# The second half of an MLP group, moved ahead of the transposes in the attention steps

## The reference, cut to what matters

```python
# attention: q, k, v are (4, 8, 576, 64)
scores = scale * np.matmul(q, k.transpose(0, 1, 3, 2))
mask = block_i >= block_j                      # blocks of 64 positions
scores = np.where(mask, scores, -1000000000.0)
scores = scores - np.max(scores, axis=-1, keepdims=True)
attn = np.exp(scores)
attn = attn / (np.sum(attn, axis=-1, keepdims=True) + 1e-09)
out = np.matmul(attn, v)
...
# dense MLP: x is (2304, 512), w_in (512, 2048), w_out (2048, 512)
h = x @ w_in
g = np.maximum(0.01 * h, h)
return (g @ w_out).astype(np.float32)
...
# routed MLP: 8 experts of 512 x 1024 and 1024 x 512, one for each token, and a skip
```

## Time and profile before

| what | value |
|---|---|
| three runs | 756.45, 757.16, 758.13 us; median 757.16 |
| the profiled execution | 757.67 us, of which the span of the trace is 755.9 |
| TensorE busy | 739.1 us, 98% |
| its weight loads busy | 595.1 us, 79% |
| Vector, Scalar, POOL engine busy | 360.1, 296.7, 146.0 us |
| chain that ended last | 92% PE, 3% DMA, 2% ACT, 2% DVE |

### The profile page before, as it was taken

How to read it: one execution, slowest core, us unless ns; L and a number is a source line. 1 busy time by engine, 2 the same in 40 slices (tenths; PEclk the granted TensorE clock), 3 DMA queues, 4 the chain that set the end, 5 groups by cost and what they waited for, 6 DMA issues and landing times.

```text
span 755.9 us, 12647 instructions
## 1 busy us (share of the span) xinstructions
PE 739.1 (98%) x4358; PEld 595.1 (79%) x4359; DVE 360.1 (48%) x761; ACT 296.7 (39%) x674; POOL 146.0 (19%) x190
## 2 busy tenths in 40 slices
PE   7999999999999999999999999999999999999997
PEld 4556777788877887797888788888787879999984
DVE  5777554465446442013435465555655352352641
ACT  5567565455445543234423222132221131342550
POOL 3136565233222221100020000000000032212221
PEclk9999999999999999999999999999999999999999
DMA  4345777545554522546756566666653117777771
GB/s 128 98 125 164 209 207 224 150 132 151 145 163 140 145 85 72 149 134 166 216 180 187 160 181 165 199 166 177 184 157 99 57 40 249 230 235 245 234 235 56
DMA packets 97537, 121.60 MB, mean 161 GB/s; under 512 B 13842, under 2 KB 60706, under 8 KB 97480
## 3 DMA queue, kind: packets, MB, share of 16 engines
q1 hardware_dynamic: 94664, 116.50, 52.8%
q0 software_dynamic: 1920, 3.77, 1.5%
q10 hardware_dynamic: 896, 0.59, 0.2%
HBM read 89.09 MB, written 31.31 MB: 159 GB/s over the span
## 4 chain that ended last, share of the span: by engine, by line
PE 92%; DMA 3%; ACT 2%; DVE 2%; issue 2%; POOL 0%; SPq 0%; DVEq 0%; POOLq 0%; ACTq 0%
PE ps_x L1809 9%; PE ps_x L1811 9%; PE ps_x L1810 9%; PE ps_h L1727 9%; PE ps_hid L1981 9%; PE ps_h L1729 8%; PE ps_h L1728 8%; PE ps_o L1710 6%; PE ps_t L1684 5%; PE ps_y L1992 2%; PE ps_y L1994 2%; PE ps_y L1993 2%; PE ps_s L1635 2%; PE ps_s L1672 2%; PE ps_s L1671 2%
## 5 line engine op out<-in xcount | busy, mean ns | idle before, releaser
L1727 PE MATMUL ps_h<-xh,win_h 128*128 128x512 f32 (+1 forms) x320 | 124.3, 388 | 5.1 <-ACT act L1083 4.9
L1729 PE MATMUL ps_h<-xh,win_l 128*128 128x512 f32 (+1 forms) x320 | 118.4, 370 | 0.0
L1728 PE MATMUL ps_h<-xl,win_h 128*128 128x512 f32 (+1 forms) x320 | 118.1, 369 | 0.0
L1809 PE MATMUL ps_x<-wout_h,g_hi 128*128 128x512 f32 x288 | 114.0, 396 | 0.0
L1811 PE MATMUL ps_x<-wout_h,g_lo 128*128 128x512 f32 x288 | 112.3, 390 | 0.0
L1810 PE MATMUL ps_x<-wout_l,g_hi 128*128 128x512 f32 x288 | 112.1, 389 | 0.0
L1069 ACT ACTIVATE prob<-ps_s,neg_max 128x128 f32<-128x128 f32 (+3 forms) x144 | 79.0, 550 | 59.5 <-DVE neg_max L1290 42.5
L1290 DVE TENSOR_REDUCE neg_max<-ps_s 128x1 f32<-128x128 f32 (+3 forms) x144 | 71.1, 509 | 58.0 <-PE ps_s L1672 36.2
L1083 ACT ACTIVATE act<-ps_h 128x512 f32<-128x512 f32 (+1 forms) x80 | 44.3, 554 | 106.3 <-PE ps_h L1729 100.0
L1330 DVE TENSOR_TENSOR g_lo<-g_raw,g_hi 128x512 fp32r<-128x512 f32 x72 | 49.5, 687 | 66.9 <-ACT g_hi L1093 66.8
L1727 PEld LDWEIGHTS ps_h<-xh,win_h 128*128 128x128 f32 x320 | 60.3, 189 | 18.2 <-issue 4.7
(11 more groups left out here) (205 smaller groups left out, 1098.5 us busy)
## 6 DMA issues: line engine op xcount, KB each, us to landing
g_raw<-hidden SPq DMA_DIRECT2D x72, 256.0 KB, 3.9
hidden<-act SPq DMA_DIRECT2D x64, 256.0 KB, 2.6
w_sb<-in_w SPq DMA_DIRECT2D x32, 512.0 KB, 5.0
w_two<-in_w SPq DMA_DIRECT2D x32, 512.0 KB, 4.6
k_raw<-in_k_t SPq DMA_DIRECT2D x40, 144.0 KB, 3.1
x2rows<-x SPq DMA_DIRECT2D x18, 256.0 KB, 2.4
out<-x SPq DMA_DIRECT2D x18, 256.0 KB, 2.6
w_stage<-in_w_in SPq DMA_DIRECT2D x16, 256.0 KB, 3.0
```

The costliest lines, as they stand in the source:

```text
L1727: e.matmul(dst, win_h[:, f, kc, :], xh[m][:, kc, :], start=kc == 0, stop=False)
L1728: e.matmul(dst, win_h[:, f, kc, :], xl[m][:, kc, :], start=False, stop=False)
L1729: last = e.matmul(dst, win_l[:, f, kc, :], xh[m][:, kc, :], start=False, stop=kc == KC - 1)
L1809: e.matmul(dst, hi, wout_h[:, f, :], start=f == 0, stop=False)
```

## The change

In the steps done one by one, a half whose `part` is 1 is issued directly behind the scores of unit s + 2. A half whose `part` is 0 stays at the step's end. Nothing else differs.

```diff
--- before.py
+++ after.py
@@ -1753,6 +1753,10 @@
             for s in range(DOUBLE):
                 if ROW_UNITS <= s + 2:
                     scores(s + 2)
+
+                for g, part in FILL[s]:
+                    if part:
+                        hidden(g, part)
                 if s >= 2:
                     transposes(s - 2)
                 products_with_v(s)
@@ -1764,7 +1768,8 @@
                     if n < GROUPS * ROW_PAIRS:
                         scores_of_both(n)
                 for g, part in FILL[s]:
-                    hidden(g, part)
+                    if not part:
+                        hidden(g, part)
```

## The result

The changed kernel takes 760.85 us, the median of 7 runs (759.36 to 762.07), against 757.29 us for the kernel before in 7 runs (756.45 to 758.65). The ratio is 1.0041 with a 95% interval of 1.0028 to 1.0054, that is 2.1 to 4.1 us slower.

What follows compares the result with a forecast made beforehand. TensorE was taken as the bound, in flight 739.1 of 755.9 us. Losses of 5.07 less gains of 1.80 made net +3.3 us on the median of 757.16, so 760.4 us, range 758.0 to 763.0.

Steps and rivals of the forecast that it cites:

- Bound, unit prices, seams: TensorE bounds; 0.23 us a product; new seams between scores and halves put at nothing, at most 1.3 us.
- The gains: Waits at the bank vanish for groups 2, 4, 5, 13 and shrink for 12, 14, 15: 1.80 us in sum.
- Steps 70, 61, 68, 55: Bank's copy, behind exponentials or turned rows, loses its cover; stalls grow by 0.98, 0.74, 0.95 and 0.80 us.
- Step 51: Bank's copy stands behind the exponential of the last scores_of_both, delaying group 1's first half: +0.85 us.
- Step 82: Unit 87's scores wait for a slot freed by an exponential that hangs on the turned inverse: +0.75 us.
- The sum: Losses 5.07 us, gains 1.80, net +3.3; what is lost stays lost behind step 86.
- B: Rival, faster: the exponential never holds up the bank's copy; 753.0, or 755.4 us with the seven gains alone; chance 0.08.
- C: Rival, no change: some of six losses are covered, most likely in steps 51 and 82; 758.0 us; chance 0.15.
- E: Rival, worse: seams cost their 1.3 us, or delayed turned rows hold up transposes; 762 to 765 us; chance 0.09.
- D: Rival: six stalls of 0.7 to 1.6 us bring TensorE's clock down, costing 15 us; 776 us; chance 0.02.

Runs made afterwards that it cites:

- the kernel with the copy first: All sixteen halves moved as in the changed kernel, plus the finished group's copy first in the Scalar engine's step; 757.16 us, ratio 0.9976 to the kernel before.
- six steps: Against the kernel before, only the second halves of steps 51, 55, 61, 68, 70 and 82 moved; 763.31 us, ratio 1.0060.
- the ten steps: Against the kernel before, second halves moved except in steps 51, 55, 61, 68, 70 and 82; 755.35 us, ratio 0.9951; again 0.9977.
- five halves ahead of the scores: Fifteen halves moved (not step 82's), group's copy first in five Scalar steps, five halves ahead of scores; against the kernel before 753.78 us, ratio 0.9942.
- the run with the copy first and step 82 as before: Changed kernel with the group's copy first in the Scalar engine's step and step 82's half left at its end; ratio 0.9986 to the kernel before.

## Why the prediction was right

Forecast 760.4, measured 760.85; forecast +3.3, measured +3.6 in the medians and +2.9 in the trace. That the time lies so close is in part luck: the stretch shows 0.4 less than the forecast's sum, and the medians' difference holds 0.6 that is not in the stretch and that no run places.

**Bound, unit prices, seams.** Right. The seams that I bounded by 0 and 1.3 us and put at nothing cost 0.15 in all, 0.05 at each of three.

**The gains.** Right. Groups 2, 4, 5 and 13 don't stall (1.27, 2.37, 2.81 and 3.67 behind the last product, all TensorE's own work), and 12, 14 and 15 stand at 1.18, 1.18 and 1.17.

**Steps 70, 61, 68, 55.** The chains were forecast at 2.37, 2.37, 2.55 and 2.66, and measured at 2.36, 2.36, 2.55 and 2.66.

**Step 51.** The mechanism is right, the term too large: 0.85 forecast, 0.64 measured. TensorE's, the Vector and the Scalar engine's timelines:

```profile
74.78 0.20 PE L1638 MATMUL ps_s<-mask_k,mask_q 64*128 64x64 bf16 x2
...
77.15 0.47 PE L1727 MATMUL ps_h<-xh,win_h 128*128 128x512 f32 x1 [0.57 <-ACT act L1083]
```

```profile
75.01 0.69 DVE L1290 TENSOR_REDUCE neg_max<-ps_s 128x1 f32<-128x512 f32 x1 [3.81 <-PE ps_s L1638]
```

```profile
75.74 0.69 ACT L1069 ACTIVATE prob<-ps_s,neg_max 128x512 f32<-128x512 f32 x1 [4.56 <-DVE neg_max L1290]
...
76.42 0.59 ACT L1083 ACTIVATE act<-ps_h 128x512 f32<-128x512 f32 x1
```

Group 1's first half comes 4.09 behind group 0's last product, and 3.45 in the kernel with the copy first, where it doesn't wait: 0.64. From the mask product to the copy it is 1.64, where I took 1.81 from the earlier trace rows. That older figure was not the chain: the copy at 73.68 waited for the second half, whose last product came then behind the scores. It is in TensorE's timeline of the kernel before, 0.42 ahead of the copy, as at the floor:

```profile
73.26 0.39 PE L1729 MATMUL ps_h<-xh,win_l 128*128 128x512 f32 x1
```

A distance between two rows is a chain's length only if nothing else ended last.

**Step 82.** Forecast +0.75; the timeline of TensorE shows the wait.

```profile
157.66 0.41 PE L1684 MATMUL ps_t<-ident,prob 128*128 128x128 f32 x2
158.59 0.39 PE L1671 MATMUL ps_s<-k_st,q_hi 128*128 128x256 f32 x1 [0.52 <-ACT prob L1069]
```

0.93 from transposes to scores. In the kernel before the transposes stood 0.17 ahead of the scores at 154.09:

```profile
153.92 0.41 PE L1684 MATMUL ps_t<-ident,prob 128*128 128x128 f32 x2
```

So it is +0.76. The chain runs as written, over the inverse's copy at 156.52, the maximum at 157.06 and the exponential at 157.76.

**The sum.** With 0.64 in place of 0.85 the terms give 3.06, and the stretch shows 2.91. By the runs with ten and with six steps the gains are 1.84 (2.08 less group 6's 0.24) where I had 1.80, and the losses 4.76 where the corrected terms have 4.86. The seams' 0.15 would come on top of the terms, so some 0.3 us of small errors stay unplaced. What was lost did stay lost, to within 1 us: behind group 16 the two profiles of the changed kernel take 596.4 and 596.3 us, the two of the kernel before 597.1 and 596.9. The eight stalled first halves that I announced are there, with 6.5 us of stalls against the 6.7 announced.

**The rivals.** B (the copy is never held up) fell, and with the copy moved first it comes true in part. C's doubt was of steps 51 and 82: both cost. E's price for seams is 0.15 and not 1.3, and no transpose waited for turned rows. D, the clock: it stayed at 1.00 in this stretch through stalls of up to 1.54 us.

## What to carry to other kernels

When filler work is moved on one engine, look at who covered whom: ask for each queue that serves the buffer's release what stands in front of the releasing instruction, and whether its source now comes behind the filler. Where a release shares an in-order queue with other work, its place must move together with the producer's; here each edit alone lost 2 to 3 us of the stretch, and both together, chosen step by step, gained 2.6. It needs doing only where the instruction in front is late: in the ten steps the filler could move alone. And sixteen moves of one kind are sixteen cases: ten gained 2.1 us, six lost 4.8.

## What the runs showed of the hardware beyond that

TensorE's clock does fall in this kernel, in some executions, far from the change. All thirteen profiles have one long stall of TensorE that ends between 317 and 328 us, with 1.38 to 2.00 us recorded as idle. Behind it the clock falls in two of them. In the second profile of the ten steps:

```profile
316.72 0.28 PE L1729 MATMUL ps_h<-xh,win_l 128*128 128x256 f32 x1
318.93 0.39 PE L1727 MATMUL ps_h<-xh,win_h 128*128 128x256 f32 x1 [1.93 <-ACT act L1083]
...
320.17 0.41 PE L1727 MATMUL ps_h<-xh,win_h 128*128 128x256 f32 x1
320.38 0.41 PE L1728 MATMUL ps_h<-xl,win_h 128*128 128x256 f32 x1
...
323.05 0.28 PE L1727 MATMUL ps_h<-xh,win_h 128*128 128x256 f32 x1
323.16 0.28 PE L1728 MATMUL ps_h<-xl,win_h 128*128 128x256 f32 x1
```

The windows of the same profile over 320 to 325 us; the granted clock is the third figure from the end.

```profile
320.00:325.00 5.00, 5.00 (x34) 5.00 (x34) 0.22 (x1) 0.77 (x2) 0.00 (x0) 0.74 0.45 127
```

From 319.1 to 322.5 products of 256 columns start 0.21 apart in place of 0.12, at the lower of the two levels (1.2 GHz; the window's mean over both levels is 0.74), which costs some 1.5 us. The other is the first profile with five halves ahead of the scores: 1.75 idle before 317.62, then products 0.21 apart to 321.10. The first profile of the kernel before has the stall at 321.20 (1.79 idle) and keeps its clock, and so does the run with the copy first and step 82 as before, with 2.00 idle, the longest of all. So the length of the stall doesn't decide it; what does stays open. Behind group 16 the two profiles with the fallen clock take 599.1 and 598.3 us, the eleven others 596.3 to 597.3.

This goes with the mean granted clock of an execution: the kernel before took 757.5 us on average in its 15 executions at 0.999 or 1.000 on one chip, and 759.3 in the 7 at 0.996 or 0.997. The ten steps' second timing had 5 of 12 executions at 0.996, averaging 757.3, against 755.1 for the 4 at 0.999; its first had none at 0.996. That is likely one reason why its two timings differ; it is argued from these means and was not tried by an experiment of its own.

By the Trainium skill, "TensorE: Matmul & The Clock Gate", in its section on psum-queue depth-cycling, short idles between groups of matmuls can make the clock swing. In the stretch of the change no run agrees: the kernel before has ten stalls of up to 0.81 us there and the changed kernel eight of up to 1.54, all at a granted clock of 1.00. The fall behind 318 us follows one long stall and not repeated short ones, so it doesn't bear that section out either.
